# Squared tiles transposed through DRAM instead of by DMAs within SBUF, in a fused attention and two-layer MoE kernel

## The chip, the cores and the metric

One core of a Trainium2 chip runs the kernel. The metric is the device time of one execution in microseconds; lower is better. The kernel before takes 496.92 us, the median of 3 runs (496.0 to 498.28).

## The reference

Three layers follow each other, all in float32:

```python
# attention: batch 2, 8 heads, 768 positions, head size 64
keep = is_sink | in_window                 # 4 sink keys, window of 128
a = softmax(where(keep, q @ k.T / 8, -1e9))
x = (a @ v)  ->  [1536, 512]
# first layer
h = x @ w_in                               # [1536, 1024]
solu = h * softmax(h)
x = layer_norm(solu) * g_ln @ w_out        # [1536, 512]
# second layer
h = x @ w_in2                              # [1536, 2048]
g = relu(h) ** 2
out = g @ w_out2                           # [1536, 512]
```

The kernel reaches float32 accuracy on the TensorE by splitting each operand into a rounded part (`_hi`) and a rest (`_lo`) and adding three products.

## The kernel before

The 1536 tokens are 12 tiles of 128 (`NT = 12`). Stage A goes tile by tile and runs attention and the first layer as a software pipeline: in step `t`, TensorE multiplies the probabilities of tile `t+1` with the values, transposes the normalized hidden tile `t` (`transpose_ln`, L1252), computes scores of tile `t+2` (L1166), the second product of the first layer for tile `t` (`project`, L1262, into the PSUM tile `x2_ps`, which is `w1_ps`), and the first product for tile `t+1` (`hidden`, L1224). The other engines do the softmax, the gate, the layer norm and the splits in the order written out for each of them.

Stage B starts when the last tile has left `hidden` and runs over 3 blocks of 512 tokens (`NB = 3`, `TB = 4` tiles each). For each of 16 slices `f` of the hidden size it computes 12 products of 512 columns (`hidden2`, L1424, into `score_ps`) and 12 for the output (`project2`, L1438). ScalarE and VectorE square and split in between.

The second layer wants its input with the features on the partitions. It is the moving operand `x2T_hi` / `x2T_lo` of `hidden2`. The way there:

- `square_x2(t)` (VectorE, L935) reads `x2_ps` and writes the SBUF tile `x2` (for the last tile `y[3]`) with the engine's transpose instruction, which transposes each block of 32 x 32 by itself. The blocks themselves stay where they are.
- `move_x2(t)` (the SyncE queue, L349) puts the blocks where they belong with 16 DMAs from SBUF to SBUF, one for each pair of a band of 32 partitions in the source and one in the destination `x2T`. Each moves 32 partitions of 4 pieces of 32 floats, 128 bytes a piece.
- `round_x2T(blk)` (ScalarE, L771) and `split_x2T(blk)` (VectorE, L1075) make `x2T_hi` and `x2T_lo` for one block of 512 tokens. `x2T_lo` lies in the same memory as `x2T`. Block 0 is done at the end of stage A, blocks 1 and 2 within block 0 of stage B, at `f = 7` and `f = 11`.

There is one buffer `x2` for all tiles but the last. So `square_x2(t)` waits until the moves of tile `t-1` have landed. In VectorE's order for step `t`, `square_x2(t-1)` stands ahead of `normalize_hidden(t)` (L894), and TensorE's `transpose_ln(t)` waits for both. The first of all squares, that of tile 0, stands in `second_step`.

The SyncE queue holds nearly all DMAs of the kernel in a written order. For `n` from 5 to 11 it is: the moves of tile `n-5`, `load_q(n)`, `load_k(n)`, `load_v(n-1)`, and for `n` below 8 one load of the second layer's weights (1 MB). For `n = 5` the load of q stands first. After the loop come the moves of tiles 7, 8 and 9, the eight loads of `w2out` (4 MB), and the moves of tiles 10 and 11. Each load waits for the buffer that it overwrites: `load_v(n-1)` for TensorE's values of tile `n-2`.

Of the kernel before, what the change touches and what calls it, by code (L numbers as in the profile page):

```python
# [13 lines left out]
F32 = mybir.dt.float32  # L14
# [6 lines left out]
P = 128  # L21
# [28 lines left out]
BLK = BANK  # L50
SQ = 32
QUADS = P // SQ
MOVES = 16 * QUADS * QUADS
NB = T // BLK
TB = BLK // P
X2T_AT = (7, 11)
# [78 lines left out]
def attention_moe_program(nc, qT, kT, v, w_in, w_out, g_ln, w2_in, w2_out, out):  # L135
# [6 lines left out]
    with ctx:  # L142
# [30 lines left out]
        def score_banks(n, p):  # L173

            return (score_pair, wt_pair)[p // 2 if alone(n) else p % 2]

        def sbt(name, shape, dt=F32):
            return ctx.enter_context(nc.sbuf_tensor(name, shape, dt))

# [29 lines left out]

        xT_hi = sa("xT_hi", [P, MC, P], F32R)  # L210
        xT_lo = sa("xT_lo", [P, MC, P], F32R)
        x2T = sa("x2T", [P, MC, T])
        w2in = sa("w2in", [P, MC, F2])
        w_hi = sa("w_hi", [P, MC, F1], F32R)
        w_lo = sa("w_lo", [P, MC, F1], F32R)
# [31 lines left out]

        relu_0 = sbt("relu_0", [P, BLK])
        sq_0 = sbt("sq_0", [P, BLK])
        x2T_lo = sbt("x2T_lo", [P, MC, T], F32R)  # L250
        w2in_lo = sbt("w2in_lo", [P, MC, F2], F32R)
        raw_stack = ExitStack()
        w2out = raw_stack.enter_context(nc.sbuf_tensor("w2out", [P, C2, DM], F32))
# [34 lines left out]
        u_ready, bstat_ready, hz_ready, hz_eps_ready = sem("u_ready"), sem("bstat_ready"), sem("hz_ready"), sem("hz_eps_ready")  # L288
        moments_ready, var_ready, ln_ready = sem("moments_ready"), sem("var_ready"), sem("ln_ready")
        z_ready, rz_ready, p_normed = sem("z_ready"), sem("rz_ready"), sem("p_normed")  # L290
        lnT_split, xT_split, x2T_moved = sem("lnT_split"), sem("xT_split"), [sem(f"x2T_moved{b}") for b in range(NB)]
        w_rounded, w_rounded_act, w_split, wo_rounded, wo_split = sem("w_rounded"), sem("w_rounded_act"), sem("w_split"), sem("wo_rounded"), sem("wo_split")
        wo_half_read = sem("wo_half_read")
        w_split_pool, wo_scaled_pool, wo_split_pool = sem("w_split_pool"), sem("wo_scaled_pool"), sem("wo_split_pool")
        exped, pT_copied, p_sinkT_copied, h_exped = sem("exped"), sem("pT_copied"), sem("p_sinkT_copied"), sem("h_exped")
        lnT_rounded, xT_rounded, x2_squared = sem("lnT_rounded"), sem("xT_rounded"), sem("x2_squared")
        x2T_rounded, x2T_split = sem("x2T_rounded"), sem("x2T_split")
        w2in_rounded, w2in_split = sem("w2in_rounded"), sem("w2in_split")
        w2out_rounded, w2out_split = sem("w2out_rounded"), sem("w2out_split")
# [3 lines left out]

        block = ctx.enter_context(nc.Block())


        def squares_of(t):

# [13 lines left out]
        @block.sync  # L322
        def _(sp):
            def load_q(n):
                if since(n, 3):
                    sp.wait_ge(q_split, n - 2)
                for half in range(2):
                    rows, heads = half_heads(half)
                    sp.dma_start(q_raw[rows, :, :], qT[n, :, heads, :]).then_inc(q_loaded, 16)

            def load_k(n):
                if since(n, 3):
                    sp.wait_ge(k_split, n - 1)
                for half in range(2):
                    rows, heads = half_heads(half)
                    sp.dma_start(k_raw[rows, :, :], kT[n, :, heads, :]).then_inc(k_loaded, 16)

            def load_v(n):
                if since(n, 2):
                    sp.wait_ge(pv_done, GROUPS * n)  # L340
                sp.dma_start(V[:, n % 2, :], v[n]).then_inc(v_loaded[n % 2], 16)

            def move_x2(t):

                sp.wait_ge(x2_squared, t + 1)
                squares = squares_of(t).rearrange("p (c r b) -> p c r b", r=QUADS, b=SQ)
                for i in range(QUADS):
                    for r in range(QUADS):
                        sp.dma_start(x2T[r * SQ:(r + 1) * SQ, :, t * P + i * SQ:t * P + (i + 1) * SQ],  # L349
                                     squares[i * SQ:(i + 1) * SQ, :, r, :]).then_inc(x2T_moved[t // TB], 16)  # L350

            def load_w_in(c):
                sp.dma_start(w_raw[:, c, :], w_in[c * P:(c + 1) * P, :]).then_inc(w_loaded[c], 16)

            def load_w_out(c):
                sp.dma_start(wo_raw[:, c * C1 // 2:(c + 1) * C1 // 2, :],
                             w_out[c * F1 // 2:(c + 1) * F1 // 2, :].rearrange("(k p) m -> p k m", p=P)
                             ).then_inc(wo_loaded[c], 16)

            def load_k01(n):  # L360
                for half in range(2):
                    rows, heads = half_heads(half)
                    sp.dma_start(k01[rows, n, :, :], kT[n, :, heads, :]).then_inc(k01_loaded[n], 16)

            def load_v_sink(b):
                sp.dma_start(v_sink_raw[0:SKS, b, :],
                             v[b * TPB, 0:N_SINK, :].unsqueeze(0).to_broadcast([SPLITS * H, N_SINK, DM])
                             ).then_inc(v_sink_loaded[b], 16)

            load_k01(0)  # L370
            load_w_in(0)
            load_w_in(1)
            load_v(0)
            load_k01(1)
            load_w_in(2)
            load_v_sink(0)
            load_w_in(3)
            load_k(2)
            load_q(2)
            load_v(1)  # L380
            load_w_out(0)
            load_w_out(1)
            load_v_sink(1)
            for n in range(3, NT):
                if n == 5:
                    load_q(n)
                if n >= 5:
                    move_x2(n - 5)
                if n != 5:
                    load_q(n)  # L390
                load_k(n)
                load_v(n - 1)
                if n == 4:
                    sp.wait_ge(w_split, MC - 1)
                    sp.wait_ge(w_split_pool, 4)
                    sp.wait_ge(wo_split, len(WO_DVE))
                    sp.wait_ge(wo_split_pool, len(WO_POOL))
                if n in range(4, 4 + MC):
                    c = n - 4
                    sp.dma_start(w2in[:, c, :], w2_in[c * P:(c + 1) * P, :]).then_inc(w2in_loaded, 16)  # L400
            move_x2(NT - 5)
            load_v(NT - 1)
            move_x2(NT - 4)
            move_x2(NT - 3)
            sp.wait_ge(h_done, 2 * NT)
            for c in range(C2 // 2):
                sp.dma_start(w2out[:, 2 * c:2 * c + 2, :],
                             w2_out[2 * c * P:(2 * c + 2) * P, :].rearrange("(c p) m -> p c m", p=P)
                             ).then_inc(w2out_loaded[c], 16)
            move_x2(NT - 2)  # L410
            move_x2(NT - 1)
            with sp.Fori(0, NB) as blk:
                for i in range(TB):

                    sp.wait_ge((y_copied_act, y_copied_dve)[i % 2], TB // 2 * blk + (i // 2 + 1))
                    sp.dma_start(out[bass.ds(blk * BLK + i * P, P), :], y[i]).then_inc(y_stored, 16)
            sp.wait_ge(y_stored, 16 * TB * NB)
# [159 lines left out]
        def _(act):  # L577
# [189 lines left out]

            def round_x2T(blk):
                cols = slice(blk * BLK, (blk + 1) * BLK)
                act.wait_ge(x2T_moved[blk], TB * MOVES)  # L770
                nc.scalar.activation(x2T_hi[:, :, cols], x2T[:, :, cols], ACT.Copy).then_inc(x2T_rounded, 1)  # L771

            def round_w2out(f):
                act.wait_ge(w2out_loaded[f // 2], 16)
# [43 lines left out]
        def _(dve):  # L818
# [111 lines left out]
            def square_x2(t):  # L930

                dve.wait_ge(x2_done, t + 1)
                if 0 < t < NT - 1:
                    dve.wait_ge(x2T_moved[(t - 1) // TB], (t - 1) % TB * MOVES + MOVES)
                nc.vector.transpose(squares_of(t), x2_ps[:, :]).then_inc(x2_squared, 1)  # L935

            def split_v_sink(b):
                low = slice(2 * SK, SKS)
# [133 lines left out]
            def split_x2T(blk):  # L1072
                cols = slice(blk * BLK, (blk + 1) * BLK)
                dve.wait_ge(x2T_rounded, blk + 1)
                nc.vector.tensor_tensor(x2T_lo[:, :, cols], x2T[:, :, cols], x2T_hi[:, :, cols].bitcast(F32),  # L1075
                                        ALU.subtract).then_inc(x2T_split, 1)

            def split_w2out(f):
                dve.wait_ge(w2out_rounded, f + 1)
# [56 lines left out]
        def _(pe):  # L1136
# [275 lines left out]
            def hidden2(blk, f, first=0, last=MC):  # L1412
                g = blk * C2 + f
                if first == 0:
                    pe.wait_ge(w2in_split, f + 1)
                    if f == 0:
                        pe.wait_ge(x2T_split, blk + 1)
                    if f >= 2 or since(blk, 1):
                        pe.wait_ge(relu_ready, g - 1)
                fs = slice(f * P, (f + 1) * P)  # L1420
                for c in range(first, last):
                    for i in range(3):
                        ws, xs = ((w2in_hi, x2T_hi), (w2in_hi, x2T_lo), (w2in_lo, x2T_hi))[i]
                        done = mm(h2_ps[f % 2], ws[:, c, fs], xs[:, c, bass.ts(blk, BLK)],  # L1424
                                  start=(c == 0 and i == 0), stop=(c == MC - 1 and i == 2))
                if last == MC:
                    done.then_inc(h2_done, 1)
# [71 lines left out]
```

## Time and profile before

| | |
|---|---|
| median of 3 runs | 496.92 us (496.0 to 498.28) |
| profiled execution, its own time | 496.89 us |
| span of the profiled execution | 495.2 us |
| TensorE (PE) busy | 483.3 us, 98% |
| VectorE (DVE) busy | 284.5 us, 57% |
| ScalarE (ACT) busy | 200.9 us, 41% |
| GpSimd (POOL) busy | 94.3 us, 19% |
| DMA queue of SyncE (q1) | 19.7% of 16 engines' span, 39,224 packets, 28.30 MB |
| packets under 512 bytes | 29,256 of 39,717 |

A span is the time from the first to the last instruction of the profiled execution; 1.7 us of its own time lie around it. PEld is TensorE's weight load, which overlaps the matmuls. The ends of matmuls are modelled and they overlap (389 ns each, issued every 227 ns), so the busy share is not a share of peak; gaps between matmuls are what can be won. SPq is the SyncE queue that issues DMAs. A bracket such as `[0.50 <-DMA x2T<-x]` says that the engine sat idle for 0.50 us just before the instruction, and what ended the idle time. L12 is line 12 of the kernel before.

### The profile page before, as it was taken

The page shows a single profiled execution, that of the slowest core. Times are in us where ns is not written, and L with a number is a line of the kernel's source. Part 1 is how long each engine was busy: PE and PEld are TensorE (multiplying, and loading weights), DVE is VectorE, ACT ScalarE, POOL GpSimd, SP SyncE. Part 2 cuts the span into 40 slices and gives each one's busy share as a digit, 9 for nine tenths or more (in the row PEclk, how much of TensorE's full clock was granted, in tenths as well). Part 3 has the DMA queues.
Part 4 walks back from the last instruction along what each step waited for, and adds up shares of the span by engine and source line. Part 5 has one row for each costly group of instructions (what it writes and reads, how often), then busy time and mean ns, then how long its engine had stood idle before and what let it go on. Part 6 is the DMA issues. An engine that isn't in the chain of part 4 may idle for free.

```text
span 495.2 us, 7334 instructions
## 1 busy us (share of the span) xinstructions
PE 483.3 (98%) x2644; PEld 392.8 (79%) x2644; DVE 284.5 (57%) x512; ACT 200.9 (41%) x531; POOL 94.3 (19%) x138
## 2 busy tenths in 40 slices
PE   7989989999999999999999999999999999999997
PEld 5667767888778888878888888888888888888885
DVE  3999888898898888775673554323222332222232
ACT  3667646545655663532334253322112221211221
POOL 2555042120022112267970000000000000000000
PEclk9999999999999999999999999999999999999999
DMA  8921343352222221119100000010000001000002
GB/s 222 309 79 43 134 106 104 124 161 64 59 60 76 53 48 34 17 30 344 29 3 0 1 0 1 34 51 0 0 0 0 0 23 63 0 1 0 0 1 85
DMA packets 39717, 29.21 MB, mean 59 GB/s; under 512 B 29256, under 2 KB 29256, under 8 KB 39176
## 3 DMA queue, kind: packets, MB, share of 16 engines
q1 hardware_dynamic: 39224, 28.30, 19.7%
q10 hardware_dynamic: 464, 0.53, 0.5%
q8 instruction: 18, 0.29, 0.2%
q14 instruction: 11, 0.09, 0.1%
HBM read 22.52 MB, written 3.15 MB: 52 GB/s over the span
## 4 chain that ended last, share of the span: by engine, by line
PE 82%; DVE 10%; SPq 2%; ACT 2%; DMA 1%; issue 1%; POOL 0%; DVEq 0%
PE score_ps L1424 26%; PE h_ps L1438 13%; PE w_ps L1262 10%; PE h_ps L1224 9%; PE wt_ps L1438 7%; PE w_ps L1438 7%; PE o_ps L1194 3%; SPq L349 2%; PE score_ps L1166 2%; PE wt_ps L1174 2%; DVE nmax L850 1%; DVE wo_lo L946 1%; PE wt_ps L1166 1%; PE h_ps L1252 1%; DMA x2T<-kT 1%; DVE prob L915 1%
## 5 line engine op out<-in xcount | busy, mean ns | idle before, releaser
L1424 PE MATMUL score_ps<-x2T_hi,w2in_hi 128*128 (+1 forms) x192 | 74.8, 389 | 0.0
L1424 PE MATMUL score_ps<-x2T_hi,w2in_lo 128*128 (+1 forms) x192 | 74.7, 389 | 0.0
L1424 PE MATMUL score_ps<-x2T_lo,w2in_hi 128*128 (+1 forms) x192 | 74.7, 389 | 0.0
L1099 DVE TENSOR_TENSOR e<-e 128x512 f32<-128x512 f32 x24 | 17.1, 712 | 82.1 <-ACT e L785 82.1
L1099 DVE TENSOR_TENSOR sq<-relu 128x512 f32<-128x512 f32 x24 | 17.7, 738 | 77.9 <-ACT relu L785 77.9
L785 ACT ACTIVATE relu<-score_ps 128x512 f32<-128x512 f32 x24 | 14.4, 598 | 94.2 <-PE score_ps L1424 94.2
L785 ACT ACTIVATE e<-score_ps 128x512 f32<-128x512 f32 x24 | 14.4, 600 | 92.5 <-PE score_ps L1424 92.5
L1424 PEld LDWEIGHTS score_ps<-x2T_hi,w2in_hi 128*128 128x128 f32 x192 | 36.1, 188 | 7.5
L1424 PEld LDWEIGHTS score_ps<-x2T_lo,w2in_hi 128*128 128x128 f32 x192 | 36.0, 188 | 7.5
L1424 PEld LDWEIGHTS score_ps<-x2T_hi,w2in_lo 128*128 128x128 f32 x192 | 36.0, 188 | 7.4
L610 ACT ACTIVATE prob<-sm,nbias 128x132 f32<-128x132 f32 (+1 forms) x96 | 37.9, 396 | 0.5
L1224 PE MATMUL h_ps<-w_hi,xT_hi 128*128 128x512 f32 x88 | 35.6, 405 | 1.3 <-DVE xT_lo L927 1.3
L1262 PE MATMUL w_ps<-wo_hi,lnT_hi 128*128 128x512 f32 x88 | 35.4, 402 | 0.5 <-DVE lnT_lo L922 0.5
L1262 PE MATMUL w_ps<-wo_lo,lnT_hi 128*128 128x512 f32 x88 | 35.2, 400 | 0.0
L1224 PE MATMUL h_ps<-w_hi,xT_lo 128*128 128x512 f32 x88 | 34.4, 391 | 0.0
L1224 PE MATMUL h_ps<-w_lo,xT_hi 128*128 128x512 f32 x88 | 34.4, 391 | 0.0
L1262 PE MATMUL w_ps<-wo_hi,lnT_lo 128*128 128x512 f32 x88 | 34.4, 391 | 0.0
L629 ACT ACTIVATE e<-h_ps,nhmax 128x512 f32<-128x512 f32 x24 | 16.3, 685 | 24.8 <-DVE nhmax L860 24.8
L572 POOL TENSOR_TENSOR w2in_lo<-w2in,w2in_hi 128x512 fp32r<-128x512 f32 x16 | 23.3, 1454 | 1.3
L1224 PEld LDWEIGHTS h_ps<-w_hi,xT_hi 128*128 128x128 f32 x88 | 16.5, 187 | 6.1 <-issue 1.1
L1262 PEld LDWEIGHTS w_ps<-wo_hi,lnT_hi 128*128 128x128 f32 x88 | 16.5, 188 | 5.4 <-DVE lnT_lo L922 1.3
L452 POOL CAST p_sink<-prob 128x64 fp32r<-128x64 f32 x10 | 2.4, 239 | 90.2 <-DVE prob L915 83.3
(182 smaller groups left out, 1105.7 us busy)
## 6 DMA issues: line engine op xcount, KB each, us to landing
w2in<-w_in SPq DMA_DIRECT2D x4, 1024.0 KB, 5.5
w2out<-w_out SPq DMA_DIRECT2D x8, 512.0 KB, 7.5
V<-v SPq DMA_DIRECT2D x12, 256.0 KB, 2.7
x2T<-x SPq DMA_DIRECT2D x176, 16.0 KB, 1.9
k_raw<-kT SPq DMA_DIRECT2D x20, 132.0 KB, 2.8
q_raw<-qT SPq DMA_DIRECT2D x20, 128.0 KB, 2.8
w2in<-w_in SPq DMA_DIRECT2D x4, 512.0 KB, 7.9
w2in<-w_out SPq DMA_DIRECT2D x2, 1024.0 KB, 13.3
```

Of the source, the lines that this page charges most:

```text
L349: sp.dma_start(x2T[r * SQ:(r + 1) * SQ, :, t * P + i * SQ:t * P + (i + 1) * SQ], squares[i * SQ:(i + 1) * SQ, :, r, :]).then_inc(x2T_moved ...
L572: nc.gpsimd.tensor_tensor(w2in_lo[:, :, fs], w2in[:, :, fs], w2in_hi[:, :, fs].bitcast(F32), ALU.subtract).then_inc(w2in_split, 1)
L610: nc.scalar.activation(prob[:, h, seen(n)], sm[:, h, seen(n)], ACT.Exp, bias=nbias[:, h:h + 1], scale=SCALE, accum_out=psum_row[:, h:h + 1 ...
L629: nc.scalar.activation(e[:, cols], h_ps[:, cols], ACT.Exp, bias=nhmax[:, :], scale=1.0, accum_out=hsum[:, half:half + 1]).then_inc(h_exped, 1)
L785: nc.scalar.activation(relu[f % 2], h2_ps[f % 2], ACT.Relu).then_inc(relu_ready, 1)
L1099: nc.vector.tensor_tensor(sq[f % 2], relu[f % 2], relu[f % 2], ALU.mult).then_inc(sq_ready, 1)
L1166: done = mm(score_banks(n, p)[:, j, cols], qs[rows], ks[rows], start=(n < 2 or i == 0), stop=(n < 2 or i == len(products) - 1))
L1194: last = mm(o_ps[rows, cols], V[:, slot, h * D:(h + 1) * D], pT[:, g, j * P:(j + 1) * P], start=(g == 0 and part == 0 and i < 2), stop=(al ...
L1224: done = mm(h_ps[:, cols], xs[:, c, :], ws[:, c, cols], start=(c == 0 and k == 0), stop=(c == MC - 1 and k == 2))
L1262: done = mm(x2_ps[:, :], ls[:, k, :], ws[:, k, :], start=(k == 0 and i == 0), stop=(k == C1 - 1 and i == 2))
L1424: done = mm(h2_ps[f % 2], ws[:, c, fs], xs[:, c, bass.ts(blk, BLK)], start=(c == 0 and i == 0), stop=(c == MC - 1 and i == 2))
L1438: done = mm(y_ps[q], gs[f % 2][:, qs], ws[:, f, :], start=(f == 0 and i == 0), stop=(f == C2 - 1 and i == 2))
```

## The change

The squared tile of 128 x 512 is written to a DRAM tensor by one DMA, and each block of 512 tokens is read back by four DMAs, one for each band of 32 partitions. For the pieces to be long, VectorE's transpose reads `x2_ps` with its 32-column groups in another order (`p r c b` in place of `p c r b`), and `x2T` and `x2T_lo` hold their free dimension as 48 groups of 32 tokens with 4 x 32 elements in each, in place of 4 rows of 1536 tokens. `x2T_hi` keeps its layout. `round_x2T` and `split_x2T` reorder between the two, and the product in `hidden2` that reads `x2T_lo` streams 16 runs of 32 columns, 512 bytes apart, in place of 512 contiguous columns. The DRAM side of the store is contiguous (2 KB a partition); each load moves 32 partitions of 16 pieces of 512 bytes.

In the queue, each move is replaced by its store at the same place. The four loads of block 0 follow the store of tile 4 (`n = 9`), those of block 1 the store of tile 8, those of block 2 the store of tile 11. `square_x2(t)` now waits for the store of tile `t-1`.

```diff
-MOVES = 16 * QUADS * QUADS
+MOVES = 16 * QUADS
...
+        x2_dram = nc.dram_tensor("x2_dram", (T // SQ, SQ, QUADS, MC * SQ), F32).ap()
...
-        x2T = sa("x2T", [P, MC, T])
+        x2T = sa("x2T", [P, T // SQ, MC * SQ])
...
-            def move_x2(t):
+            def store_x2(t):
 
                 sp.wait_ge(x2_squared, t + 1)
-                squares = squares_of(t).rearrange("p (c r b) -> p c r b", r=QUADS, b=SQ)
-                for i in range(QUADS):
-                    for r in range(QUADS):
-                        sp.dma_start(x2T[r * SQ:(r + 1) * SQ, :, t * P + i * SQ:t * P + (i + 1) * SQ],
-                                     squares[i * SQ:(i + 1) * SQ, :, r, :]).then_inc(x2T_moved[t // TB], 16)
+                sp.dma_start(x2_dram[t * QUADS:(t + 1) * QUADS, :, :, :].rearrange("s c r e -> (s c) (r e)"), squares_of(t)
+                             ).then_inc(x2_stored, 16)
+
+            def load_x2T(blk):
+
+                sp.wait_ge(x2_stored, 16 * TB * (blk + 1))
+                squares = slice(blk * TB * QUADS, (blk + 1) * TB * QUADS)
+                for r in range(QUADS):
+                    sp.dma_start(x2T[r * SQ:(r + 1) * SQ, squares, :], x2_dram[squares, :, r, :].rearrange("s c e -> c s e")
+                                 ).then_inc(x2T_loaded[blk], 16)
...
                 if n >= 5:
-                    move_x2(n - 5)
+                    store_x2(n - 5)
+                if n >= 5 and (n - 5) % TB == 0 and n > 5:
+                    load_x2T((n - 5) // TB - 1)
...
-            move_x2(NT - 5)
+            store_x2(NT - 5)
             load_v(NT - 1)
-            move_x2(NT - 4)
-            move_x2(NT - 3)
+            store_x2(NT - 4)
+            load_x2T(1)
+            store_x2(NT - 3)
             sp.wait_ge(h_done, 2 * NT)
...
-            move_x2(NT - 2)
-            move_x2(NT - 1)
+            store_x2(NT - 2)
+            store_x2(NT - 1)
+            load_x2T(2)
...
-                nc.scalar.activation(x2T_hi[:, :, cols], x2T[:, :, cols], ACT.Copy).then_inc(x2T_rounded, 1)
+                nc.scalar.activation(x2T_hi[:, :, cols].rearrange("p c (s b) -> p c s b", b=SQ), chunked(x2T, blk), ACT.Copy
+                                     ).then_inc(x2T_rounded, 1)
...
                 if 0 < t < NT - 1:
-                    dve.wait_ge(x2T_moved[(t - 1) // TB], (t - 1) % TB * MOVES + MOVES)
-                nc.vector.transpose(squares_of(t), x2_ps[:, :]).then_inc(x2_squared, 1)
+                    dve.wait_ge(x2_stored, 16 * t)
+                nc.vector.transpose(squares_of(t), x2_ps[:, :].rearrange("p (c r b) -> p r c b", r=QUADS, b=SQ)
+                                    ).then_inc(x2_squared, 1)
...
-                        ws, xs = ((w2in_hi, x2T_hi), (w2in_hi, x2T_lo), (w2in_lo, x2T_hi))[i]
-                        done = mm(h2_ps[f % 2], ws[:, c, fs], xs[:, c, bass.ts(blk, BLK)],
+                        high = x2T_hi[:, c, bass.ts(blk, BLK)]
+                        low = x2T_lo[:, bass.ts(blk, TB * QUADS), c * SQ:(c + 1) * SQ]
+                        ws, xs = ((w2in_hi, high), (w2in_hi, low), (w2in_lo, high))[i]
+                        done = mm(h2_ps[f % 2], ws[:, c, fs], xs,
                                   start=(c == 0 and i == 0), stop=(c == MC - 1 and i == 2))
```

## Rows read from the trace of the kernel before

**Rows 1.** Busy time by window: length, busy (x instructions) of five engines, clock, DMA, GB/s.

```profile
70.00:224.00 154.00, 151.78 (x1040) 124.01 (x1040) 129.08 (x272) 84.36 (x280) 36.21 (x61) 1.00 0.29 77
224.00:492.00 268.00, 267.79 (x1185) 221.27 (x1183) 95.97 (x127) 75.76 (x123) 30.50 (x27) 1.00 0.07 25
```

**Rows 2.** Waits of PE from 70 us on: in total, times, longest.

```profile
PE w_ps L1252 <- DVE u L894: 1.3, 2, 0.9
```

**Rows 3.** Chain that ended last, the pieces ahead of 70 us: start, length, what.

```profile
57.70 1.30 SPq L349
68.09 1.84 DMA x2T<-x
```

**Rows 4.** Timeline around tile 1's square: start, length, engine, line, instruction, [idle before].

```profile
69.36 0.16 DVE L882 TENSOR_TENSOR var<-moments,hz_eps 128x1 f32<-128x1 f32 x1
69.61 0.55 POOL L471 TENSOR_TENSOR rstd<-var,minus_half 128x1 f32<-128x1 f32 x1 [0.48 <-DVE var L882]
...
69.77 0.66 PE L1211 MATMUL o_ps<-p_sinkT,v_sink 96*128 96x128 f32 x4
...
70.03 0.72 DVE L935 STREAM_TRANSPOSE x<-w_ps 128x512 f32<-128x512 f32 x1 [0.50 <-DMA x2T<-x]
...
70.67 0.96 DVE L894 TENSOR_SCALAR u<-u,moments,rstd 128x512 f32<-128x512 f32 x2
...
71.32 0.41 PE L1252 MATMUL w_ps<-ident,u 128*128 128x128 f32 x2 [0.89 <-DVE u L894]
```

**Rows 5.** Timeline at the same place of the next step.

```profile
87.44 0.70 DVE L935 STREAM_TRANSPOSE x<-w_ps 128x512 f32<-128x512 f32 x1
...
88.20 1.00 DVE L894 TENSOR_SCALAR u<-u,moments,rstd 128x512 f32<-128x512 f32 x2
88.39 0.52 PEld L1211 LDWEIGHTS o_ps<-p_sinkT,v_sink 96*128 96x128 f32 x4 [0.17 <-issue]
...
88.86 0.20 PEld L1252 LDWEIGHTS w_ps<-ident,u 128*128 128x128 f32 x2
```

**Rows 6.** Timeline of the SyncE queue, moves of tiles 1 and 4, loads behind them.

```profile
71.12 11.34 SPq L349 DMA_DIRECT2D x2T<-x  x16
...
122.92 10.71 SPq L349 DMA_DIRECT2D x2T<-x  x16
133.68 1.24 SPq L329 DMA_DIRECT2D q_raw<-qT  x2
...
220.92 5.23 SPq L407 DMA_DIRECT2D w2out<-w_out  x8
```

**Rows 7.** Timeline of ScalarE, the rounding of q for tile 9.

```profile
137.05 0.64 ACT L601 ACTIVATE QH<-q_raw 128x512 fp32r<-128x512 f32 x1
```

**Rows 8.** DMA issues by line: count, KB each, median us from issue to landing.

```profile
q_raw<-qT SPq DMA_DIRECT2D x20, 128.0 KB, 2.8
...
out<-x SPq DMA_DIRECT2D x3, 256.0 KB, 2.1
```

**Rows 9.** Groups by line and shape: count, busy us, mean ns, idle before.

```profile
L1075 DVE TENSOR_TENSOR x2T_lo<-x2T,x2T_hi 128x2048 fp32r<-128x2048 f32 x3 | 7.2, 2412 | 2.9 <-ACT x2T_hi L771 2.9
...
L935 DVE STREAM_TRANSPOSE x<-w_ps 128x512 f32<-128x512 f32 x11 | 7.8, 709 | 0.8 <-DMA x2T<-x 0.5 <-PE w_ps L1262 0.3
...
L771 ACT ACTIVATE x2T_hi<-x2T 128x2048 fp32r<-128x2048 f32 x3 | 5.7, 1907 | 0.0
...
L831 DVE TENSOR_TENSOR sm<-wt_ps,alone_mask 128x512 f32<-128x512 f32 x2 | 1.4, 686 | 0.0
```

**Rows 10.** Timeline of VectorE after the first split of `x2T`.

```profile
218.75 0.69 DVE L855 TENSOR_REDUCE hmax<-h_ps 128x1 f32<-128x512 f32 x1 [0.50 <-PE h_ps L1224]
```

**Rows 11.** Timeline of TensorE, score products of 260 columns.

```profile
72.54 0.28 PE L1166 MATMUL score_ps<-KL,QH 64*128 64x260 f32 x2
72.66 0.28 PE L1166 MATMUL score_ps<-KH,QL 64*128 64x260 f32 x2
```

**Rows 12.** Chain that ended last, one slice of `hidden2` in stage B.

```profile
238.66 2.72 PE score_ps L1424 x12
```

More of the change, by code:

```diff
@@ L249, in attention_moe_program @@
         sq_0 = sbt("sq_0", [P, BLK])
-        x2T_lo = sbt("x2T_lo", [P, MC, T], F32R)
+        x2T_lo = sbt("x2T_lo", [P, T // SQ, MC * SQ], F32R)
         w2in_lo = sbt("w2in_lo", [P, MC, F2], F32R)
@@ L290, in attention_moe_program @@
         z_ready, rz_ready, p_normed = sem("z_ready"), sem("rz_ready"), sem("p_normed")
-        lnT_split, xT_split, x2T_moved = sem("lnT_split"), sem("xT_split"), [sem(f"x2T_moved{b}") for b in range(NB)]
+        lnT_split, xT_split, x2_stored = sem("lnT_split"), sem("xT_split"), sem("x2_stored")
         w_rounded, w_rounded_act, w_split, wo_rounded, wo_split = sem("w_rounded"), sem("w_rounded_act"), sem("w_split"), sem("wo_rounded"), sem("wo_split")
@@ L296, in attention_moe_program @@
         lnT_rounded, xT_rounded, x2_squared = sem("lnT_rounded"), sem("xT_rounded"), sem("x2_squared")
+        x2T_loaded = [sem(f"x2T_loaded{b}") for b in range(NB)]
         x2T_rounded, x2T_split = sem("x2T_rounded"), sem("x2T_split")
@@ L304, in attention_moe_program, with chunked @@
         block = ctx.enter_context(nc.Block())
+        def chunked(x, blk):
+            return x[:, blk * TB * QUADS:(blk + 1) * TB * QUADS, :].rearrange("p s (c b) -> p c s b", b=SQ)
         def squares_of(t):
@@ L769, in round_x2T @@
                 cols = slice(blk * BLK, (blk + 1) * BLK)
-                act.wait_ge(x2T_moved[blk], TB * MOVES)
-                nc.scalar.activation(x2T_hi[:, :, cols], x2T[:, :, cols], ACT.Copy).then_inc(x2T_rounded, 1)
+                act.wait_ge(x2T_loaded[blk], MOVES)
+                nc.scalar.activation(x2T_hi[:, :, cols].rearrange("p c (s b) -> p c s b", b=SQ), chunked(x2T, blk), ACT.Copy
+                                     ).then_inc(x2T_rounded, 1)
             def round_w2out(f):
@@ L1074, in split_x2T @@
                 dve.wait_ge(x2T_rounded, blk + 1)
-                nc.vector.tensor_tensor(x2T_lo[:, :, cols], x2T[:, :, cols], x2T_hi[:, :, cols].bitcast(F32),
-                                        ALU.subtract).then_inc(x2T_split, 1)
+                high = x2T_hi[:, :, cols].rearrange("p c (s b) -> p c s b", b=SQ)
+                nc.vector.tensor_tensor(chunked(x2T_lo, blk), chunked(x2T, blk), high.bitcast(F32), ALU.subtract
+                                        ).then_inc(x2T_split, 1)
             def split_w2out(f):
```

## The prediction

> **What bounds the kernel now.** I read the windows first, for which engine fills each stage. From 224 us to the end TensorE has work for 267.8 of 268 us, at the full clock (1.00 granted, the 2.4 GHz level) [rows 1]. Nothing that arrives earlier can shorten that stretch; only a longer matmul can change it. From 70 to 224 us TensorE is busy for 151.8 of 154 us [rows 1], so 2.2 us are to be had there at the most. The waits of TensorE say which they are: the largest is the transposition of the normalized tile (L1252) waiting for VectorE's `u`, 1.3 us in two places, 0.9 us in one of them [rows 2]. Then the chain, read backwards from the end: stage B, then TensorE through most of stage A, and at 70 us it leaves the compute engines. It goes through a DMA `x2T<-x` that lands at 69.93 us and into SyncE's issue of the sixteen moves of tile 0, which begins at 57.70 [rows 3]. This is the one place where the removed work stands on the path.
>
> The timeline shows it in detail [rows 4]. VectorE finishes `var` at 69.52 and could start the square of tile 1, but the sixteenth move of tile 0 lands only at 69.93, since SyncE needs about 11 us to issue sixteen DMAs (11.34 and 10.71 us for tiles 1 and 4) [rows 6]. It idles for 0.50 us, squares at 70.03, normalizes at 70.67, and TensorE, which had finished its previous matmuls at 70.43, idles for 0.89 us until 71.32. One step later the same sequence shows no wait: square 87.44, `u` 88.20, TensorE's next weights 88.86 directly behind those of the sinks [rows 5]. For every other tile the buffer `x2` is free long before it is wanted: the moves of tile 1 are issued from 71.12 to 82.46 [rows 6] and the next square is at 87.44 [rows 5].
>
> **Removed: the moves on SyncE.** 12 tiles x 16 DMAs = 192 issues at 10.7 to 11.3 us a tile [rows 6] are some 130 us of queue time. In their place stand 12 stores and 12 loads. A store writes the same 256 KB as an output store, which lands 2.1 us after issue [rows 8]. The store of tile 0 goes out at 57.70 and lands near 60 us, some 9 us ahead of need. Even behind other traffic it would have to take 11.7 us to be late. So VectorE's 0.50 us goes. What is late next: the square would run from about 69.55 to 70.25, and `rstd` from GpSimd is there at 70.16 [rows 4], so `u` starts 0.45 to 0.5 us earlier, and TensorE, free since 70.43, resumes at about 70.84 rather than 71.32. It still waits 0.4 us, for VectorE's own work. **Term: -0.5 us.** It is carried to the end, because everything later hangs on TensorE's order or on chains that start from its results.
>
> **Queue effects behind that.** Each q load stood behind a move, in the worst cases 11 us. Without it the loads start earlier, bounded by their own buffer waits. The v loads wait for TensorE's values and don't move. What could be hurt is what stands behind the new loads: at `n = 9` the four loads of block 0 precede the q load of tile 9. A q load of 128 KB, in pieces of 512 bytes as well, lands in 2.8 us [rows 8]. Four loads of 256 KB, each twice as large, are at most 4 x 2 x 2.8 = 22 us if nothing overlapped, and 5 to 6 us if they pipeline. I take the second, since sixteen moves in flight overlap too. They start at about 123.5 us where the move of tile 4 started at 122.92; before, the q load went out at 133.68 [rows 6] and ScalarE needed it at 137.05 [rows 7]. New: issued by 127, landed by 134 at the latest. **Term: 0**, with 3 us of cover. If it all serialized, ScalarE would start its step up to 9 us late, once.
>
> The `w2out` loads went out at 220.92 because the queue still held moves [rows 6]; they now go out as soon as `hidden` of the last tile is done, somewhat earlier. Their first user waits for a product of TensorE. Term 0. The stores of tiles 10 and 11 and the loads of block 2 end near 250 us. Their user stands at `f = 11` of block 0: 224 us plus 12 slices of twice 2.72 us [rows 12] is about 289 us. Term 0, with 39 us of cover.
>
> **Changed: VectorE's square.** The instruction has the same 512 columns, but reads PSUM in 16 runs of 32. It takes 709 ns contiguous, and an add of 128x512 that reads PSUM in four runs of 128 takes 686 ns [rows 9], no more than the transpose. So breaks cost nothing where a row shows them. I take 0. The lower bound is also 0, since the column count stays; the upper bound, twice the time, is a rival below, because this instruction has almost no cover: `u`'s first half ends near 88.70, and TensorE wants it at 88.86 [rows 5]. The margin is 0.16 us.
>
> **Changed: round and split of `x2T`.** 1.9 us and 2.3 to 2.7 us for 2048 columns [rows 9], now with runs of 32. For block 0 VectorE idles for 0.50 us right after the split [rows 10], and in stage B TensorE is ahead anyway. Term 0; up to 0.5 us more is free.
>
> **Changed: the `x2T_lo` operand.** 192 of the 576 products of `hidden2` stream 16 runs of 32 columns. Twelve contiguous products take 2.72 us, 0.227 us each [rows 12], or 0.443 ns a column. No row shows a moving operand with gaps. Lower bound 0. For the upper bound I let each break cost what a new instruction costs: score products of 260 columns, two side by side, follow each other in 0.12 us [rows 11] against 260 x 0.443 = 0.115 us, so 5 ns. 15 breaks x 5 ns x 192 = 14.4 us. I take 0, the end that VectorE's reads with breaks point to. By one column time a break the cost would be 15 x 0.443 x 192 = 1.3 us, which I keep in the range.
>
> On operands with gaps the Trainium skill has a rule (SBUF — State Buffer, section "Door 1: The DMA port swizzle", the note on cachelines): reads of SBUF are full speed while consecutive accesses stay within 16-byte lines. Runs of 128 bytes use all of each line, so by it the matmul stays at 0. The same note says that any non-contiguous access pattern in PSUM significantly slows matmuls down; it speaks against this change if it also holds for VectorE's read of `x2_ps`, which is the first rival. Taken as a matter of 8-byte lines it wouldn't, since 128-byte runs fill those as well. No run here shows which reading is right.
>
> **Sum.** 496.9 (profiled execution, own time) - 0.5 = 496.4 us. The median of the runs shown is 496.92, so against it the forecast is 496.4 as well, 0.1% less. A measurement of this kernel can tell about 0.5%, 2.5 us, from no change.
>
> **Rivals.**
>
> 1. *The square becomes slower (slower).* Against it speaks the row of the add; for it, that this transposing instruction was never seen with a source in pieces. Nine squares (tiles 1 to 9) stand ahead of a normalization that TensorE waits for. At two of them, the two waits of [rows 2], VectorE is already the later one; at the other seven it has 0.16 us. Doubled (+0.70 us): 2 x 0.70 + 7 x 0.54 = 5.2 us; with the gain of 0.5, 501.6 us. It starts to cost at +0.16 us and is a measurable loss from about +0.46 us. Chance 7%.
>
> 2. *The operand with gaps slows TensorE (slower).* At the upper bound 496.4 + 14.4 = 510.8 us. TensorE is the bound of stage B, so each ns a break is 2.9 us of time; measurable from 1 ns, about two columns. Against it: nothing in the trace, only the analogy with VectorE. Chance 7%.
>
> 3. *The gain doesn't come.* GpSimd's `rstd` at 70.16, or a store that takes over 11.7 us, takes the place of the DMA: 496.9 us. For it: `rstd` ends only 0.1 us before it would be wanted. Chance 9%.
>
> 4. *More goes than expected.* The freed queue and 192 fewer transfers take away all of TensorE's waits for VectorE of [rows 2], 1.3 us, and another 0.6 us of the 2.2 us that TensorE is idle from 70 to 224 us [rows 1]: 495.0 us. Chance 4%. Even all 2.2 us of idle time after 70 us would not be a measurable gain.
>
> The forecast, 496.4, gets 70%; 3% are left for a larger gain by a mechanism that no row shows.
>
> **Range and chances.** Low end 495.0, rival 4. High end 499.0: forecast plus 1.3 us for one column a break, plus the 1.4 us by which the highest run shown lies above the median. The rest of rivals 1 and 2 stays out. Faster by over 0.5%: those 3%. Within 0.5%: 84%, the forecast, rivals 3 and 4, and 1% for mild forms of rivals 1 and 2. Slower: 13%, the rest of rivals 1 and 2.
>
> **What the profile after would show.** `L935` without idle time before it at 70 us, `u` at about 70.2, TensorE resuming near 70.8; the chain no longer passing through SyncE. The square at 0.70 us and the normalization at the same distance behind `var` as in [rows 5]. Twelve products of `hidden2` still in 2.72 us, also those of `x2T_lo`. The q load of tile 9 landed before 136 us. If the matmuls on `x2T_lo` are spaced wider than 0.227 us, or the square is above 0.86 us, the prediction is wrong and the sign with it.

## The result, and the profile after

The changed kernel takes 499.73 us (median of 5 runs, 499.17 to 499.98); the kernel before takes 496.92 us beside it. The ratio is 1.0059, 95% interval 1.0042 to 1.0076: slower by 0.6%, 2.8 us. The forecast was 496.4 us.

| | before | after |
|---|---|---|
| profiled execution, its own time | 496.89 us | 499.17 us |
| span | 495.2 us | 497.4 us |
| TensorE busy | 483.3 us | 486.0 us |
| VectorE busy | 284.5 us | 286.0 us |
| packets of the SyncE queue | 39,224 | 19,640 |
| DRAM written | 3.15 MB | 6.29 MB |

**The gain came where it was forecast.** The first view is the timeline of the changed kernel around the square of tile 1, beside [rows 4]. Lines have moved: the square is L952, `var` L899, the normalization L911, the transposition L1271.

```profile
69.00 0.16 DVE L899 TENSOR_TENSOR var<-moments,hz_eps 128x1 f32<-128x1 f32 x1
69.11 0.72 DVE L952 STREAM_TRANSPOSE x<-w_ps 128x512 f32<-128x512 f32 x1
69.24 0.55 POOL L487 TENSOR_TENSOR rstd<-var,minus_half 128x1 f32<-128x1 f32 x1 [0.48 <-DVE var L899]
...
70.52 0.41 PE L1271 MATMUL w_ps<-ident,u 128*128 128x128 f32 x2 [0.45 <-DVE u L911]
```

VectorE no longer idles ahead of the square (no bracket on L952), and TensorE waits for 0.45 us in place of 0.89. The start of the kernel differs by a microsecond or so from one execution to the next, so I measure from the square of tile 0, at 56.43 before (first line) and 56.05 after:

```profile
56.43 0.71 DVE L935 STREAM_TRANSPOSE x<-w_ps 128x512 f32<-128x512 f32 x1
...
56.05 0.71 DVE L952 STREAM_TRANSPOSE x<-w_ps 128x512 f32<-128x512 f32 x1
```

From there to the square of tile 1 it is 13.60 us before [rows 4] and 13.06 us after: 0.54 us won by VectorE. The term of 0.5 was TensorE's, though: its transposition starts 71.32 - 56.43 = 14.89 us behind tile 0's square before and 70.52 - 56.05 = 14.47 after, so 0.42 us are won there, against 0.48 in the prediction's working. Of these, 0.36 us are left when stage B starts (below). The transposing instruction itself takes as long as before, 708 ns against 709 [rows 9], although it now reads PSUM in runs of 32. The reordering of round and split cost nothing either (by groups, mean ns after the bar):

```profile
L952 DVE STREAM_TRANSPOSE x<-w_ps 128x512 f32<-128x512 f32 x11 | 7.8, 708 | 0.3 <-PE w_ps L1281 0.3
L1094 DVE TENSOR_TENSOR x2T_lo<-x2T,x2T_hi 128x2048 fp32r<-128x2048 f32 x3 | 7.2, 2414 | 2.9 <-ACT x2T_hi L787 2.9
L787 ACT ACTIVATE x2T_hi<-x2T 128x2048 fp32r<-128x2048 f32 x3 | 5.7, 1909 | 0.0
```

**The loss is in stage B.** There TensorE was said to be the bound, and only a longer matmul could change it. The chain of the kernel before shows 12 products of `hidden2` in 2.72 us [rows 12]; the chain of the changed kernel (start, length, what), with the first stretch of stage B and two later slices:

```profile
223.41 4.18 PE score_ps L1445 x18
...
282.10 2.79 PE score_ps L1445 x12
...
287.61 2.79 PE score_ps L1445 x12
```

A slice of 24 products takes 287.61 - 282.10 = 5.51 us. Before it is 5.44 us:

```profile
224.15 4.09 PE score_ps L1424 x18
...
282.35 2.72 PE score_ps L1424 x12
...
287.79 2.72 PE score_ps L1424 x12
```

The mean over 28 slices late in stage B, taken from the starts of the matmuls, is 5.507 against 5.440 us. That is 67 ns a slice, or 16.7 ns for each of its four products with `x2T_lo`, and 48 x 0.067 = 3.2 us in all. To check this I take stage B from its start to where the chain leaves TensorE for the last time:

```profile
491.82 0.69 DVE y L1111
...
494.11 0.69 DVE y L1130
```

It is 491.82 - 224.15 = 267.67 us before and 494.11 - 223.41 = 270.70 after, 3.0 us more. The missing 0.2 us is nearly all a delay of 0.15 us that the kernel before had in one slice and the changed kernel has not (before, then after):

```profile
257.70 0.83 PE wt_ps L1438 x3
...
257.35 0.68 PE wt_ps L1459 x3
```

From tile 0's square to the start of stage B it is 167.72 before and 167.36 after, 0.36 us less. The groups by form show that longer matmuls aren't only those that read in pieces (mean ns after the bar):

```profile
L1445 PE MATMUL score_ps<-x2T_lo,w2in_hi 128*128 x128 | 51.1, 399 | 0.0
L1445 PE MATMUL score_ps<-x2T_hi,w2in_lo 128*128 x128 | 50.5, 395 | 0.0
L1445 PE MATMUL score_ps<-x2T_hi,w2in_hi 128*128 x128 | 50.1, 391 | 0.0
```

All three were at 389 ns before:

```profile
L1424 PE MATMUL score_ps<-x2T_lo,w2in_hi 128*128 x128 | 49.8, 389 | 0.0
```

The product with `x2T_lo` is 10 ns longer, the one behind it 6 ns, though that one reads 512 contiguous columns. The ends of matmuls are modelled, so these lengths are a hint; the period of the slice is the measurement.

**The queue** did as forecast. These are its issues and their landings after the change (count, KB each, median us to landing):

```profile
x2T<-x_dram SPq DMA_DIRECT2D x12, 256.0 KB, 5.1
x_dram<-x SPq DMA_DIRECT2D x11, 256.0 KB, 3.3
...
x_dram<-y SPq DMA_DIRECT2D x1, 256.0 KB, 2.0
```

A store lands in 3.3 us, not in the 2.1 us of an output store [rows 8]; the prediction had allowed it 11.7. That most stores stand right behind other loads is the likely reason: the last one (`y`), issued with no load shortly ahead of it, lands in 2.0 us. The four loads of block 0 are issued in 2.3 us, and the q load behind them at 127.16 in place of 133.68 [rows 6]:

```profile
122.64 2.26 SPq L361 DMA_DIRECT2D x2T<-x_dram  x4
127.16 1.11 SPq L336 DMA_DIRECT2D q_raw<-qT  x2
...
218.00 4.82 SPq L422 DMA_DIRECT2D w2out<-w_out  x8
```

ScalarE rounds that q at 136.28 us, without a wait.

### The profile page after: what moved, and what is told of

Same layout as the page of the kernel before. It is cut to its first block, busy times and chain, and to the rows that moved or that the text cites. A ratio compares the mean times of both kernels' runs of the same rounds, so it can differ in the third digit from the quotient of the medians.

```text
span 497.4 us, 7166 instructions
## 1 busy us (share of the span) xinstructions
PE 486.0 (98%) x2644; PEld 393.1 (79%) x2644; DVE 286.0 (57%) x512; ACT 200.2 (40%) x531; POOL 93.8 (19%) x138
## 3 DMA queue, kind: packets, MB, share of 16 engines
q1 hardware_dynamic: 19640, 31.43, 21.1%
HBM read 25.66 MB, written 6.29 MB: 64 GB/s over the span
## 4 chain that ended last, share of the span: by engine, by line
PE 83%; DVE 10%; ACT 3%; DMA 2%; issue 1%; SPq 1%; POOL 0%; DVEq 0%; ACTq 0%
PE score_ps L1445 27%; PE h_ps L1459 13%; PE w_ps L1281 10%; PE h_ps L1243 10%; PE w_ps L1459 7%; PE wt_ps L1459 7%; PE o_ps L1213 3%; DMA x2T<-kT 2%; PE score_ps L1185 2%; PE wt_ps L1193 1%; PE wt_ps L1185 1%; PE h_ps L1271 1%; DVE prob L932 1%; DVE bstat L889 1%; PE o_ps L1230 1%
## 5 line engine op out<-in xcount | busy, mean ns | idle before, releaser
L1445 PE MATMUL score_ps<-x2T_lo,w2in_hi 128*128 (+1 forms) x192 | 76.6, 399 | 0.0
L1445 PE MATMUL score_ps<-x2T_hi,w2in_lo 128*128 (+1 forms) x192 | 75.8, 395 | 0.0
L802 ACT ACTIVATE relu<-score_ps 128x512 f32<-128x512 f32 x24 | 14.4, 598 | 95.7 <-PE score_ps L1445 95.7
L802 ACT ACTIVATE e<-score_ps 128x512 f32<-128x512 f32 x24 | 14.4, 599 | 94.0 <-PE score_ps L1445 94.0
L661 ACT ACTIVATE xT_hi<-o_ps 128x512 fp32r<-128x512 f32 x12 | 7.2, 598 | 30.9 <-PE o_ps L1230 28.7
```

The costliest lines, as they stand in the source:

```text
L661: nc.scalar.activation(xT_hi[:, :, :], o_ps[:, :].rearrange("p (c q) -> p c q", q=P), ACT.Copy).then_inc(xT_rounded, 1)
L802: nc.scalar.activation(relu[f % 2], h2_ps[f % 2], ACT.Relu).then_inc(relu_ready, 1)
L1445: done = mm(h2_ps[f % 2], ws[:, c, fs], xs, start=(c == 0 and i == 0), stop=(c == MC - 1 and i == 2))
```

## The experiments

Theory A: the operand with gaps is the whole loss. Theory B: the DRAM route is. Ratios are against the kernel before, beside which each ran; the intervals are 95%.

### Each part alone

**e1, the layout without the DRAM route:**

```diff
-                        sp.dma_start(x2T[r * SQ:(r + 1) * SQ, :, t * P + i * SQ:t * P + (i + 1) * SQ],
+                        sp.dma_start(x2T[r * SQ:(r + 1) * SQ, t * QUADS + i, :].rearrange("p (c b) -> p c b", b=SQ),
                                      squares[i * SQ:(i + 1) * SQ, :, r, :]).then_inc(x2T_moved[t // TB], 16)
...
+                        low = x2T_lo[:, bass.ts(blk, TB * QUADS), c * SQ:(c + 1) * SQ]
```

(and the reordering in round and split, as in the change)

> The new layout of x2T and x2T_lo alone: the sixteen moves a tile within SBUF stay, VectorE's transpose reads PSUM as before, but the moves write groups of 32 tokens and hidden2 streams x2T_lo in 16 runs of 32. Theory A (the operand with gaps is the whole loss): 12 products of hidden2 in 2.79 us as in the change, and VectorE idle before tile 1's square again, so 496.9 + 3.4 = 500.3 us. Theory B (the loss comes with the DRAM route, not with the operand): 2.72 us and 496.9 us.

Measured: 499.07 us, ratio 1.0054 (1.0040 to 1.0068). In the chain:

```profile
281.91 2.79 PE score_ps L1432 x12
...
287.42 2.79 PE score_ps L1432 x12
```

The loss is there without any DRAM traffic. Theory B falls. It is 1.2 us less than expected. Of that, 0.3 us is the kernel before, which measured 496.56 us beside this run, and 0.2 us the operand, which costs 3.2 us and not 3.4. Another 0.5 us shows in the trace: VectorE did not wait for the moves of tile 0 in this execution. Its square of tile 1 starts at 69.03 without idle time, 13.10 us behind that of tile 0.

```profile
55.93 0.71 DVE L940 STREAM_TRANSPOSE x<-w_ps 128x512 f32<-128x512 f32 x1
...
57.20 10.50 SPq L353 DMA_DIRECT2D x2T<-x  x16
...
69.03 0.72 DVE L940 STREAM_TRANSPOSE x<-w_ps 128x512 f32<-128x512 f32 x1
...
139.48 11.37 SPq L353 DMA_DIRECT2D x2T<-x  x16
```

Tile 0's sixteen issues took 10.50 us, against 10.99 before:

```profile
57.70 10.99 SPq L349 DMA_DIRECT2D x2T<-x  x16
```

These moves write 512 contiguous bytes a partition in place of four pieces of 128, but that isn't shown to be the reason. Over the first eight tiles the issues took 10.50 to 11.37 us here and 10.71 to 11.34 before, 11.0 and 11.1 in the mean. So the 0.5 us of the forecast stood on an edge: half a microsecond of issue time decides it, and two tiles of one execution differ by more than that. With one trace of each kernel I can't tell how often the kernel before pays it.

**e2, the DRAM route without the layout.** The DRAM tensor is laid out by feature, the stores scatter pieces of 128 bytes, and the loads read 2 KB pieces into a contiguous `x2T`:

```diff
+        x2_dram = nc.dram_tensor("x2_dram", (SQ, QUADS, MC, T), F32).ap()
...
+                squares = squares_of(t).rearrange("p (e b) -> p e b", b=SQ)
+                for i in range(QUADS):
+                    sp.dma_start(x2_dram[:, :, :, t * P + i * SQ:t * P + (i + 1) * SQ].rearrange("p r c b -> p (r c) b"),
+                                 squares[i * SQ:(i + 1) * SQ, :, :]).then_inc(x2_stored, 16)
...
+                for r in range(QUADS):
+                    sp.dma_start(x2T[r * SQ:(r + 1) * SQ, :, cols], x2_dram[:, r, :, cols]).then_inc(x2T_loaded[blk], 16)
```

(and `x2T`, `x2T_lo`, round, split and the product as in the kernel before)

> The DRAM route with x2T, x2T_lo and x2T_hi all contiguous as before: the scatter of 128-byte pieces is in the store (four DMAs a tile to DRAM), the loads read 2 KB pieces. VectorE's transpose reads PSUM in runs of 32 as in the change. Theory A: 2.72 us for 12 products, no idle time before tile 1's square, 496.9 - 0.5 = 496.4 us. Theory B: as slow as the change, 499.7 us, with 2.79 us for 12 products.

Measured: 496.32 us, ratio 0.9995 (0.9986 to 1.0004). The forecast of the change, 496.4 us, is met by this version of it. The 12 products are back at their time, and the wait before tile 1's square is gone:

```profile
69.79 0.72 DVE L948 STREAM_TRANSPOSE x<-w_ps 128x512 f32<-128x512 f32 x1
...
282.24 2.72 PE score_ps L1438 x12
...
287.68 2.72 PE score_ps L1438 x12
```

It is no measurable gain over the kernel before.

**e4, runs of 512: the changed kernel with one operand contiguous.** The product takes 512 neighbouring elements of the same block. They are not the columns that the rest term needs; the amount of work is the same.

```diff
-                        low = x2T_lo[:, bass.ts(blk, TB * QUADS), c * SQ:(c + 1) * SQ]
+                        flat_lo = x2T_lo[:, bass.ts(blk, TB * QUADS), :].rearrange("p s e -> p (s e)").rearrange("p (c e) -> p c e", c=MC)
+                        low = flat_lo[:, c, :]
```

> The changed kernel, but the product with x2T_lo streams 512 contiguous elements of the same block, which are not the right ones (the columns of the rest term are mixed up, the work is the same). Theory A: 499.7 - 3.4 = 496.3 us and 2.72 us for 12 products. Theory B: 499.7 us.

Measured: 496.88 us, ratio 1.0004 (0.9991 to 1.0016), 2.72 us for 12 products. The loss goes with one access pattern in one instruction of the source.

**e3, all three products in pieces:**

```diff
-                        high = x2T_hi[:, c, bass.ts(blk, BLK)]
+                        high = x2T_hi[:, bass.ts(blk, TB * QUADS), c * SQ:(c + 1) * SQ]
```

(and `x2T_hi`, with its rounding and its use in the split, in the layout of `x2T`)

> The changed kernel with x2T_hi in the layout of x2T as well, so that all 576 products of hidden2 stream 16 runs of 32. Theory A, each such product 17.5 ns longer: 384 more of them, 499.7 + 6.7 = 506.4 us, 12 products in 2.93 us. A rival within it (the cost arises only where a contiguous stream follows a broken one or the other way round): about 499.7 us or less. Theory B: 499.7 us.

Measured: 504.12 us, ratio 1.0150 (1.0135 to 1.0166). The price per product was expected to hold, 506.4 us, and it did not. More of the cause gives more of the effect, but three times the streams don't give three times the cost: a slice takes 289.83 - 284.24 = 5.59 us.

```profile
284.24 2.84 PE score_ps L1445 x12
...
289.83 2.84 PE score_ps L1445 x12
```

That is 12 ns for each of 12 products, against 16.7 ns for each of 4.

### What it is about the pieces

Theory A1: each break between pieces costs the same. A2: the second level of the access pattern costs a fixed time. The following kernels change the same line and read, from the same 2048 elements of the block, pieces of another length (again other columns than the rest term needs, and the same amount of work); a run of length L starts every 4 L elements. For L = 64:

```diff
-                        low = x2T_lo[:, bass.ts(blk, TB * QUADS), c * SQ:(c + 1) * SQ]
+                        flat_lo = x2T_lo[:, bass.ts(blk, TB * QUADS), :].rearrange("p s e -> p (s e)").rearrange("p (g e) -> p g e", e=256)
+                        low = flat_lo[:, :, c * 64:(c + 1) * 64]
```

> The changed kernel with the x2T_lo operand read in 64 runs of 8 elements (32 bytes) out of the same 2048 elements of the block; the wrong columns, the same amount of work. Theory A1 (each break costs the same): 63 breaks in place of 15, 17.5 x 63 / 15 = 73 ns a product, 496.3 + 14.1 = 510.4 us, 12 products in 3.01 us. Theory A2 (a fixed cost of an operand with a second level, whatever the runs): 499.4 us and 2.79 us.

> As the last, with 32 runs of 16 elements. A1: 31 breaks, 36 ns a product, 496.3 + 6.9 = 503.2 us, 12 products in 2.86 us. A2: 499.4 us and 2.79 us.

> As the last, with 8 runs of 64 elements. A1: 7 breaks, 8 ns a product, 496.3 + 1.6 = 497.9 us, 12 products in 2.75 us. A2: 499.4 us and 2.79 us.

> As the last, with 4 runs of 128 elements. A1: 3 breaks, 3.5 ns a product, 496.3 + 0.7 = 497.0 us, 12 products in 2.73 us. A2: 499.4 us and 2.79 us.

| operand | runs in a product | median us | ratio (interval) | 12 products, us | slice, us |
|---|---|---|---|---|---|
| 512 contiguous (e4) | 1 | 496.88 | 1.0004 (0.9991 to 1.0016) | 2.72 | 5.44 |
| runs of 128 | 4 | 496.61 | 0.9997 (0.9988 to 1.0007) | 2.72 | 5.44 |
| runs of 64 | 8 | 496.37 | 0.9988 (0.9971 to 1.0004) | 2.72 | 5.44 |
| runs of 32 (the change) | 16 | 499.73 | 1.0059 (1.0042 to 1.0076) | 2.79 | 5.51 |
| runs of 16 | 32 | 500.70 | 1.0083 (1.0066 to 1.0099) | 2.78 | 5.53 |
| runs of 8 | 64 | 499.82 | 1.0073 (1.0056 to 1.0091) | 2.76 | 5.51 |

The slice is the distance of two starts in the chain; for runs of 64, of 16 and of 8:

```profile
281.82 2.72 PE score_ps L1446 x12
...
287.26 2.72 PE score_ps L1446 x12
```

```profile
283.05 2.78 PE score_ps L1446 x12
...
288.57 2.78 PE score_ps L1446 x12
```

```profile
282.22 2.76 PE score_ps L1446 x12
...
287.73 2.76 PE score_ps L1446 x12
```

The 12 products don't show the whole cost where the slice grows by more than they do: the rest falls on the products of `project2` behind them. With runs of 8 it also moves within `hidden2`. There the product in pieces is 390 ns long, 1 ns more than a contiguous one, and the product ahead of it in each group of three, which reads contiguous columns, 395:

```profile
L1446 PE MATMUL score_ps<-x2T_hi,w2in_hi 128*128 x128 | 50.5, 395 | 0.0
...
L1446 PE MATMUL score_ps<-x2T_lo,w2in_hi 128*128 x128 | 49.9, 390 | 0.0
```

Both A1 and A2 fall. Down to runs of 64 the gaps are free; between 64 and 32 the cost appears at once, and with four times as many breaks it is no larger. It isn't a price for each piece; it looks like a limit that is either kept or not, though runs of 16, 87 ns a slice in place of 67, don't fit even that.

Three more kernels ask what the limit hangs on. In the change, length and step changed together; here they are parted:

```diff
-                        low = x2T_lo[:, bass.ts(blk, TB * QUADS), c * SQ:(c + 1) * SQ]
+                        flat_lo = x2T_lo[:, bass.ts(blk, TB * QUADS), :].rearrange("p s e -> p (s e)")
+                        half = flat_lo.rearrange("p (h g e) -> p h g e", h=2, e=2 * 64)[:, c // 2]
+                        low = half[:, :, c % 2 * 64:(c % 2 + 1) * 64]
```

(for runs of 32 with step 64 the same with 32; for step 0 `flat_lo[:, c * 32:(c + 1) * 32].unsqueeze(1).to_broadcast([P, BLK // SQ, SQ])`)

> The changed kernel with the x2T_lo operand read in 8 runs of 64 elements that start 128 elements (512 bytes) apart, as the runs of 32 of the change do; the wrong columns, the same amount of work. Runs of 64 that start 256 elements apart cost nothing (2.72 us for 12 products, 496.4 us), runs of 32 that start 128 apart cost 17 ns a product. Theory R (what costs is a run shorter than 64, or equally more than 7 breaks): free, 2.72 us, 496.4 us. Theory S (what costs is a step of 512 bytes or less): 2.79 us, 499.4 us.

Measured: 496.77 us, ratio 1.0001 (0.9988 to 1.0015), 2.72 us for 12 products.

> The same with 16 runs of 32 elements that start 64 elements (256 bytes) apart. Theory R: as the change, 2.79 us, 499.4 us. Theory S: costs too, but then as the runs of 16 with the same step did (2.78 us, period of a slice 5.53 us), about 500.5 us.

Measured: 500.06 us, ratio 1.0068 (1.0041 to 1.0095), 2.79 us for 12 products and 5.51 us a slice, as the change.

> The same with 16 runs of the same 32 elements, read again and again (step 0). Theory M (the cost arises in the memory, where a run leaves the stretch that it was in): less or none, 2.72 us, 496.4 us. Theory G (the cost arises in stepping the access pattern, whatever the address): 2.79 us, 499.4 us.

Measured: 499.51 us, ratio 1.0061 (1.0044 to 1.0078). Sixteen readings of the same 32 elements give the same lengths as the change, to the nanosecond:

```profile
L1446 PE MATMUL score_ps<-x2T_lo,w2in_hi 128*128 x128 | 51.1, 399 | 0.0
...
L1446 PE MATMUL score_ps<-x2T_hi,w2in_lo 128*128 x128 | 50.5, 395 | 0.0
...
L1446 PE MATMUL score_ps<-x2T_hi,w2in_hi 128*128 x128 | 50.0, 391 | 0.0
```

Neither the step nor the place of the pieces makes a difference in these kernels. Theories S and M fall, R and G stand: as far as tested, the pattern itself is what costs, not the place in the memory that it leads to.

**e7, the neighbours.** The three products of each `c` in another order, so that the ones in pieces stand in pairs:

```diff
-                    for i in range(3):
+                    for i in ((0, 2, 1) if c % 2 == 0 else (1, 0, 2)):
```

> The changed kernel with the three products of each c in another order, so that the products with x2T_lo stand in pairs; the sum is the same. With one broken stream in three a slice takes 5.51 us in place of 5.44 (17 ns a broken stream), with three in three 5.59 us (12 ns). If a part of the cost arises only where a contiguous stream follows a broken one (about 5.5 ns, by these two), pairs halve that part: a slice of 5.50 us, 0.5 us less in all, 498.9 us. If it arises in the stream alone: 5.51 us and 499.4 us.

Measured: 499.33 us, ratio 1.0064 (1.0045 to 1.0083); by total time it can't be told from the change. The slice can:

```profile
282.65 2.77 PE score_ps L1445 x12
...
288.14 2.77 PE score_ps L1445 x12
```

5.49 us (mean of 28: 5.493) against 5.51 (5.507). Paired, a stream in pieces costs 13.3 ns in place of 16.7. So the neighbours matter. That a part of the cost lies in the change from one kind of stream to the other is the likely reading, not a shown one: the order of the weights changed as well, and no run has this order with contiguous operands. Nor do two such parts add up simply: with 10 ns in the stream and 6.7 ns for each change, from these two kernels, e3 should cost 127 ns a slice, and it costs 147.

**e8, length or number?** At 512 columns a run of 32 always goes with 16 runs. These two cut the product into two of 256 columns:

```diff
+                        if i == 1:
+                            flat_lo = x2T_lo[:, bass.ts(blk, TB * QUADS), :].rearrange("p s e -> p (s e)")
+                            for part in range(2):
+                                low = flat_lo.rearrange("p (h g e) -> p h g e", h=2, e=4 * SQ)[:, part, :, c * SQ:(c + 1) * SQ]
+                                mm(h2_ps[f % 2][:, part * 256:(part + 1) * 256], w2in_hi[:, c, fs], low,
+                                   start=False, stop=False)
...
```

(for the contiguous halves `low = flat_lo[:, (2 * c + part) * 256:(2 * c + part + 1) * 256]`, other columns than the rest term needs)

> The changed kernel with each product of x2T_lo cut into two of 256 columns, both contiguous (the wrong columns, the same amount of work). It is the reference for the next one. 4 more instructions a slice: if a cut costs as little as the gap between a 260-column pair and its columns (5 ns), 2.74 us for the 12, and about 497.4 us.

> The same two halves, each in 8 runs of 32 elements, 128 elements apart. Runs of 64 were free and runs of 32 cost 17 ns a product of 512 columns, but with 512 columns a length of 64 goes with 8 runs and a length of 32 with 16. Theory L (the length of the run decides): at least half of the 17 ns in each half, so a slice 0.07 us longer than with contiguous halves, 3.4 us in all. Theory N (the number of runs in an instruction decides, 8 are free): no difference from contiguous halves.

Measured: 499.83 us (ratio 1.0049, 1.0030 to 1.0068) and 499.76 us (1.0053, 1.0037 to 1.0069), both with a slice of 5.51 us. This says less than it should. The contiguous halves cost 17 ns a product themselves, where 5 were expected. Each half loads its weights again, 384 loads in place of 192:

```profile
L1447 PEld LDWEIGHTS score_ps<-x2T_lo,w2in_hi 128*128 128x128 f32 x384 | 72.1, 188 | 16.5
```

Whether these loads are the cost is open. Their length alone doesn't say so, for in the same trace one load of 188 ns starts 0.11 us behind another:

```profile
284.09 0.19 PEld L1447 LDWEIGHTS score_ps<-x2T_lo,w2in_hi 128*128 128x128 f32 x1
284.20 0.19 PEld L1450 LDWEIGHTS score_ps<-x2T_hi,w2in_lo 128*128 128x128 f32 x1
```

What stands out is that a cut into two contiguous halves costs the same 67 ns a slice as 16 runs of 32 with any step and as 64 runs of 8, and that halves in runs cost no more. The cost of the pieces may be hidden behind that of the cut, or be of one kind with it. No difference is what theory N expected, but this reference was not clean, and I don't count it as a decision.

## Why the prediction was wrong

- **The bound** was read rightly: stage B is TensorE's alone, and only a longer matmul could lengthen it. It did.
- **Removed, the moves on SyncE:** right. -0.5 us forecast; 0.42 us of TensorE's time at the place, 0.36 us by the start of stage B. But in e1's execution the same wait was absent with the moves kept, so a part of this gain may be a matter of which execution was traced.
- **Queue effects:** right, term 0. The q load of tile 9 was on time, and the trace shows no engine waiting for a store or for a load of block 0, 1 or 2.
- **VectorE's square, round and split:** right, term 0. 708 ns with runs of 32 from PSUM. Rival 1 didn't happen.
- **The `x2T_lo` operand** is the step that failed. "I take 0, the end that VectorE's reads with breaks point to": it is 16.7 ns a product, 3.2 us in all, inside the bounds of 0 and 14.4 us. No row showed a matmul reading in pieces, and I carried over what rows of another engine showed. The sum with the measured term is 496.9 - 0.5 + 3.2 = 499.6 us, and 499.73 were measured. Matmuls spaced wider than 0.227 us were also the sign of being wrong that the prediction named. It was rival 2, in a form between its ends: 1.1 ns a break if shared out over 15 breaks, but the kernels with runs of 64 and of 8 show that sharing it out so is wrong.
- **The range** ended at 499.0 because I let only one column time a break into it, 1.3 us, beside the 1.4 us between runs (the sum is 499.1), and gave the rest of rival 2 to the 13% left out. With bounds of 0 and 14.4 us and no row near either end, the high end should have reached further, and rival 2 should have had more than 7%: it acted on the only engine without slack, 192 times.
- **The rule of the Trainium skill** on operands with gaps (SBUF — State Buffer, section "Door 1: The DMA port swizzle", note on cachelines), from which the prediction worked out that runs of 128 bytes stay at full speed, doesn't agree with the runs: 128 bytes a run cost 16.7 ns a product, 256 bytes a run nothing, and a step of 0, which never leaves the same 128 bytes, costs as much as any. Its sentence that any non-contiguous pattern in PSUM slows matmuls down was not tested for matmuls here; VectorE's read of PSUM in runs of 32 cost nothing.

Open is the mechanism behind the limit between 64 and 32, and whether it is the length of a run or the number of runs in one instruction. Why the kernel with runs of 16 is the slowest of the series, 5.53 us a slice, and why a cut into two contiguous halves costs as much as runs of 32, is open too.

## What to carry to other kernels

When a data movement off the critical path is made cheaper by a new layout, follow the layout to the last reader: here 130 us of queue time and 20,000 packets were worth 0.4 to 0.5 us, while 16.7 ns on an operand of the busiest engine, 192 times, cost 3.2 us. If a matmul operand must be read in pieces, test the piece length in the kernel: at 512 columns, runs of 64 elements (4 bytes each) were free, runs of 32 were not. An edit on an engine with no slack, of a kind that no row shows, deserves a rival with a real chance, however harmless its nearest relatives on other engines look.

## What the runs showed of the hardware

- A moving operand of 512 fp32r columns (4 bytes each) read in runs of 64 or 128 streamed as fast as a contiguous one (12 products in 2.72 us). In runs of 32 a product cost 16.7 ns more, of 16 about 22 ns, of 8 again 16.7 ns. The distance of runs of 32 made no difference: starting 128, 64 and 0 elements apart, each 5.51 us a slice.
- The cost shows at the neighbours too: the contiguous product behind one in pieces was 395 ns long in place of 389, and an order with the ones in pieces in pairs made a slice 13 ns shorter.
- Cutting a product of 512 columns into two of 256, all contiguous, cost 17 ns as well (5.51 us a slice).
- VectorE's 32x32 transpose reads PSUM in 16 reordered runs of 32 in the same 708 ns.
- Sixteen DMAs of 16 KB between bands of SBUF took 10.50 to 11.37 us to issue with 512-byte destination runs and 10.71 to 11.34 us with 128-byte ones (first eight tiles): no difference beyond the spread.
